# Second matrix chain: output also from seven products of halves, with sums made in PSUM

## The reference

```python
def _moe_ref(x, w_in, w_out):
    h = np.maximum(x @ w_in, 0.0)
    return (h * h @ w_out).astype(np.float32)      # this is y below

def _moe2_ref(x, w1, w2, w3, w_out):
    a = x @ w1                                     # 512 -> 1024
    b = x @ w2
    h = a * b @ w3                                 # 1024 -> 1024
    return (h @ w_out).astype(np.float32)          # 1024 -> 512
```

## Time and profile before

| | |
|---|---|
| median of 3 runs | 1226.66 us (1224.62 to 1226.89) |
| profiled execution | 1226.94 us, span 1225.2 us |
| TensorE busy | 1216.7 us, 99% |
| VectorE busy | 787.5 us, 64% |
| ScalarE busy | 479.3 us, 39% |
| DMA | 183.27 MB, mean 150 GB/s |
| mean granted clock of TensorE | 0.999 |

### The profile page before, as it was taken

The page is one execution under the profiler, slowest core; times in us unless marked ns, Lnnn a source line. Parts: engine busy times, 40 slices in busy tenths (PEclk is TensorE's granted clock), DMA queues, the critical chain, the costliest instruction groups (busy, mean ns, idle before and its releaser), DMA issues.

```text
span 1225.2 us, 16114 instructions
## 1 busy us (share of the span) xinstructions
PE 1216.7 (99%) x5842; PEld 1015.1 (83%) x5842; DVE 787.5 (64%) x1242; ACT 479.3 (39%) x867; POOL 75.5 (6%) x108
## 2 busy tenths in 40 slices
PE   9999999999999999999999999999999999999999
PEld 6677878888888888888888988888888888888888
DVE  6877868677786866667544667656664666465541
ACT  6666555555565554445444431121113111311110
POOL 0001112021121200000000000000000000000000
PEclk9999999999999999999999999999999999999999
DMA  9967664354445422122121463525442554343302
GB/s 316 340 237 254 216 221 138 122 172 139 148 138 176 130 86 94 60 86 69 65 72 51 183 250 137 180 95 223 146 155 95 224 182 153 118 166 137 120 1 86
DMA packets 57613, 183.27 MB, mean 150 GB/s; under 512 B 5200, under 2 KB 6736, under 8 KB 53456
## 3 DMA queue, kind: packets, MB, share of 16 engines
q1 hardware_dynamic: 45088, 137.90, 32.2%
q0 software_dynamic: 12464, 44.57, 10.5%
HBM read 128.97 MB, written 53.48 MB: 149 GB/s over the span
## 4 chain that ended last, share of the span: by engine, by line
PE 97%; DVE 1%; DMA 0%; issue 0%; ACT 0%; SPq 0%; DVEq 0%; ACTq 0%
PE ps_y L700 55%; PE ps_h L700 26%; PE ps_t L700 14%; PE ps_h L761 1%; PE ps_t L724 1%; PE ps_y L761 0%; DMA raw<-in_w_T 0%; PE ps_t L761 0%; DVE v_lo L1256 0%; DVE t L1346 0%; SPq L536 0%; DVE X_lo L1256 0%; DVE stage L1364 0%; SPq L530 0%; ACT v_hi L1006 0%
## 5 line engine op out<-in xcount | busy, mean ns | idle before, releaser
L1006 ACT CAST v_hi<-t 128x512 fp32r<-128x512 f32 (+1 forms) x176 | 106.0, 602 | 407.3 <-DVE t L1256 396.0
L700 PE MATMUL ps_y<-v_hi,X_hi 128*128 128x512 f32 (+1 forms) x576 | 219.2, 380 | 0.3 <-DVE v_lo L1256 0.3
L700 PE MATMUL ps_y<-v_lo,X_hi 128*128 128x512 f32 (+1 forms) x576 | 217.8, 378 | 0.0
L700 PE MATMUL ps_y<-v_hi,X_lo 128*128 128x512 f32 (+1 forms) x576 | 217.7, 378 | 0.0
L1256 DVE TENSOR_TENSOR t<-t 128x512 f32<-128x512 f32 (+1 forms) x208 | 135.9, 666 | 92.9 <-ACT t L1104 92.3
L1256 DVE TENSOR_TENSOR v_lo<-t,v_hi 128x512 fp32r<-128x512 f32 (+1 forms) x176 | 117.5, 668 | 79.3 <-ACT v_hi L1006 69.8
L1104 ACT ACTIVATE t<-ps_h 128x512 f32<-128x512 f32 (+1 forms) x144 | 82.7, 574 | 151.2 <-PE ps_h L700 150.6
L1256 DVE TENSOR_TENSOR t<-t,ps_y 128x512 f32<-128x512 f32 x112 | 76.2, 687 | 76.8 <-PE ps_y L700 76.1
L700 PEld LDWEIGHTS ps_y<-v_hi,X_lo 128*128 128x128 f32 x576 | 108.5, 188 | 20.3
L700 PEld LDWEIGHTS ps_y<-v_hi,X_hi 128*128 128x128 f32 x576 | 108.7, 189 | 20.0 <-issue 0.7
L700 PEld LDWEIGHTS ps_y<-v_lo,X_hi 128*128 128x128 f32 x576 | 108.7, 189 | 19.4
(11 more groups left out here) (255 smaller groups left out, 2273.7 us busy)
## 6 DMA issues: line engine op xcount, KB each, us to landing
top<-s_scratch SPq DMA_DIRECT2D x16, 1792.0 KB, 7.3
s_odd<-s_scratch SPq DMA_DIRECT2D x16, 1792.0 KB, 7.3
raw<-g_scratch SPq DMA_DIRECT2D x64, 256.0 KB
raw<-in_moe_w_in SPq DMA_DIRECT2D x32, 256.0 KB
raw<-in_x_T SPq DMA_DIRECT2D x32, 256.0 KB
raw<-in_x_tok SPq DMA_DIRECT2D x32, 256.0 KB
y_scratch<-stage POOLq DMA_DIRECT2D x8, 1024.0 KB, 6.4
s_scratch<-top POOLq DMA_DIRECT2D x32, 256.0 KB, 3.0
```

The lines of the kernel that those rows point to most:

```text
L700: mm = nc.tensor.matmul(dst, w, m, start=first and n == 0, stop=last and n == 2)
L1006: return nc.scalar.copy(dst, src)
```

## The change

The sums are made of W as well: tiles 5 and 6 get the `S_part` that tiles 1 to 4 have, now on W, and its results go to a new scratch `w_scratch`. W is no longer resident; its seven sums (1.05 MB each) are loaded for every double tile (`load_W`) into three buffers in turn: those of parts 0 to 2 behind the load of chunk 2's sums, those of parts 3 to 6 during the output phase, each when the part three before it is done.

A double tile is now eight chunks one behind the other, without output chunks between them, and then an output phase of seven parts (`out_part`), each 2 x 4 x 3 matmuls of 512 columns: halves of the outputs, of the inner 1024 and of the tokens. v stays in float32 (`e_raw`) over the whole double tile. Sets 1 to 6 of the tokens' side of the output are sums of v (`T_v_pair`, `set_src`) that are split in the output phase, two halves at a time; set 0 is split during the chunks.

In chunks and output alike the order of the products is now 0, 1, 3, 2, 4, 6, 5, and the last three are not added by VectorE: VectorE writes u4 and u3 into the PSUM banks of products 5 and 7, and the last three products are accumulated there onto P1, u4 and u3 (`start` is false for them, `p >= 4`). TensorE waits before them until P1 is copied out, u4 is written, and c22 is read. Per chunk this leaves VectorE u2, u4, u3, c22 and the two multiplications, and gives ScalarE three copies (P1, P5, c11).

The token sets' work of the next double tile (`set_round`, `set_lower`) moves into the output phase between the sets of v. The output is stored in four pieces of 0.5 MB. The remainder's last product takes W from four further loads at the end.

The diff, cut to its core:

```diff
+    w_dram = nc.dram_tensor("w_scratch", [KINDS, P, 4, 2, H], F32, kind="Internal").ap()
...
+        seq = (0, 1, 3, 2, 4, 6, 5)
+        P1_bank, P6_bank, P7_bank, P5_bank = range(4)
+        bank_of = (P1_bank, P6_bank, P5_bank, P7_bank, P1_bank, P5_bank, P7_bank)
...
+        U2, U4, U3, C22, V1, V0, REST = range(1, 8)
...
+        def set_src(p, k, n=2):
+
+            if p in (1, 6):
+                return T24_v[:, k:k + n, :]
+            if p == 2:
+                return T1_rows(k, n)
+            h, s = {0: (0, 0), 3: (0, 1), 4: (1, 0), 5: (1, 1)}[p]
+            return v_rows(h, s, k, n)
...
+        out_of = (0, 1, 3, 2, 0, 3, 2)
...
+            def load_W(t, p):
+                c = N_SETS * t + p
+                if c >= 3:
+                    sp.wait_ge(out_prod, out_count(0, c - 3))
+                sp.dma_start(W_buf(c).bitcast(F32), w_dram[seq[p]].rearrange("p k s n -> p (k s n)")
+                             ).then_inc(W_loaded[c % 3], 16)
...
+                if m == 1:
+                    for p in range(3, N_SETS):
+                        load_W(t - 1, p)
                 load_S(n)
-                t, m = n // KG, n % KG
+                if m == 2:
+                    for p in range(3):
+                        load_W(t, p)
                 if m == 2 and t < TILES - 1:
                     load_y(t + 1)
...
+            def ab_part(n, p):
+
                 t, m = n // KG, n % KG
-                pe.wait_ge(S_loaded[n % 2], 16 * (n // 2 + 1))
...
+                if p == 4:
                     pe.wait_ge(P1_copied, n + 1)
-                else:
-                    pe.wait_ge(prod_used, products_before(n) + used_at[j])
+                if p == 5:
+                    pe.wait_ge(prod_used, used_before(n) + U4)
+                if p == 6:
+                    pe.wait_ge(prod_used, used_before(n) + C22)
+                for kk in range(2):
+                    mm = product(ab_bank(n, bank_of[p]), S_buf[n % 2][:, j, kk, 0], S_buf[n % 2][:, j, kk, 1],
+                                 B_hi[j][:, kk], B_lo[j][:, kk], kk == 0 and p < 4, kk == 1, p >= 4)
+                mm.then_inc(prod_done, 1)
...
-            def out_chunk(t, half, m):
-                pe.wait_ge(ab_split, 2 * (KG * t + m) + half + 1)
...
-                w_hi, w_lo = G(m)
-                for o in range(KM):
-                    cols = slice(o * P, (o + 1) * P)
-                    last = product(out_bank(t, half, o), w_hi[:, cols], w_lo[:, cols], *v_part(half, m),
-                                   m == 0, m == KG - 1)
-                last.then_inc(out_acc, 1)
...
+            def out_part(t, p):
+
+                c = N_SETS * t + p
+                pe.wait_ge(W_loaded[c % 3], 16 * (c // 3 + 1))
...
+                for o in range(2):
+                    if p == 4:
+                        pe.wait_ge(out_P1_copied, 2 * t + o + 1)
+                    if p == 5:
+                        pe.wait_ge(out_u4, 2 * t + o + 1)
+                    if p == 6:
+                        pe.wait_ge(c22_staged, 2 * t + o + 1)
+                    for k in range(4):
+                        if o == 0 and p == 0:
+                            pe.wait_ge(B11_ready, 4 * t + k + 1)
+                        elif o == 0 and k % 2 == 0:
+                            pe.wait_ge(v_set_ready, 2 * ((N_SETS - 1) * t + p - 1) + k // 2 + 1)
+                        w = W_in(c)[:, k]
+                        cols = slice(o * P, (o + 1) * P)
+                        last = product(out_acc_bank(out_of[p], o), w[:, 0, cols], w[:, 1, cols],
+                                       set_part(p, 0, k, 1)[:, 0], set_part(p, 1, k, 1)[:, 0],
+                                       k == 0 and p < 4, k == 3, p >= 4)
+                    last.then_inc(out_prod, 1)
...
-                add(u3, u2, 2)
-                add(u4, u2, 3)
...
+                add(ab_bank(n, P5_bank), u2_in, P5_bank)
+                if between is not None:
+                    between()
+                dve.wait_ge(prod_done, base + 4)
+                add(ab_bank(n, P7_bank), u2_in, P7_bank)
+                dve.wait_ge(prod_used, used + U3)
+                add(c22_in, p5_in, P7_bank)
...
-                for half in range(2):
-                    hi, lo = v_part(half, m)
-                    minus(lo, v_new[half], hi, ab_hi, 2 * n + half + 1, ab_split)
...
+            def out_phase(t):
+                def v_set(p):
+                    for half in range(2):
+                        k = 2 * half
+                        minus(set_part(p, 1, k), set_src(p, k), set_part(p, 0, k), v_set_hi,
+                              2 * ((N_SETS - 1) * t + p - 1) + half + 1, v_set_ready)
...
+            first_block(5, S, slot5, h_of(6, S), slot6, (2, 0))
+            first_block(6, S, slot6, h_of(7, S), tile7_slot, (2, 1))
```

More of the change, by code:

```diff
@@ L577, in _ @@
                 tile(2 * i + 2, tile_slots, R_1 + PT, i, 1)
-            for b in range(NB - 3, NB - 1):
-                tile(b, tile_slots, R_1 + (b - 1) * PT)
+            sp.wait_ge(wp_stored, 16 * 2)
+            for kk in range(2):
+                for n, piece in enumerate(flat(tile_slots)):
+                    load_piece(R_1 + (4 + kk) * PT + n, piece, 5 + kk)
+                    if n == 3:
+                        sp.wait_ge(S_split, 2 * 2 * KINDS + kk * KINDS + 1)
+                        for dst, row, col in ((A11, 0, 0), (A12, 0, 1), (A21, 1, 0), (A22, 1, 1)):
+                            sp.dma_start(dst.rearrange("p (e n) -> p e n", e=2), W_block(kk, row, col)
+                                         ).then_inc(A_loaded, 16)
             tile(7, tile7_slots, R_7)
@@ L695, in passes, with product @@
                 return (w_hi, m_hi), (w_hi, m_lo), (w_lo, m_hi)
-            def product(dst, w_hi, w_lo, m_hi, m_lo, first, last):
+            def product(dst, w_hi, w_lo, m_hi, m_lo, first, last, onto=False):
                 for n, (w, m) in enumerate(passes(w_hi, w_lo, m_hi, m_lo)):
-                    mm = nc.tensor.matmul(dst, w, m, start=first and n == 0, stop=last and n == 2)
+                    mm = nc.tensor.matmul(dst, w, m, start=first and n == 0, stop=last and n == 2,
+                                          skip_group_check=onto)
                 return mm
@@ L973, in first_ab @@
                     pe.wait_ge(relu_done, KF * SR + KF)
-                    ab_chunk(0)
+                    for p in range(3):
+                        ab_part(0, p)
             h0 = batch_h(0, 0, g0_ready)
@@ L993, in _ @@
             first_block(SR, NT, sread_h, no_wait, no_wait, first_ab)
+            for p in range(3, N_SETS):
+                ab_part(0, p)
+            pe.wait_ge(y_drained_act, 2 * (SR + 1))
+            pe.wait_ge(y_drained_dve, 2 * (SR + 1))
             for t in range(TILES):
@@ L1214, in second_block @@
                         ab_chunk(KG * t + m)
[L1215 to L1219 removed]
+                out_phase(t)
             act.wait_ge(g_stored[0], stored(0, STEPS))
@@ L1478, in ab_chunk @@
-                tt(v_new[1], c22, c12, ALU.mult).then_inc(ab_done, 1)
-                for half in range(2):
-                    hi, lo = v_part(half, m)
-                    minus(lo, v_new[half], hi, ab_hi, 2 * n + half + 1, ab_split)
+                dve.wait_ge(prod_done, base + 6)
+                dve.wait_ge(prod_used, used + C22)
+                if t > 0 and m < 2:
+                    dve.wait_ge(v_set_ready, 2 * (N_SETS - 1) * t)
+                tt(v_f(m, 1), c22_in, ab_bank(n, P5_bank), ALU.mult).then_inc(prod_used, 1)
```

503 lines of the change are left out of this document (315 added, 188 removed).

## The result

The changed kernel takes 1229.52 us (median of 11 runs, 1228.25 to 1232.16) against 1225.04 us (11 runs, 1224.62 to 1226.89): ratio 1.0034, 95% interval 1.0025 to 1.0043, 4.5 us slower. The prediction was 1231.2 us. With more runs the median of the kernel before moved from 1226.66 to 1225.04 us; the profiled execution of before, at 1226.94, was one of its slower ones (1.5 us of it lie in the first two tiles, where the changed kernel's trace is that much shorter).

The account below looks back on a forecast made before the run. TensorE was taken to bound the kernel and never wait in the double tiles. From 1226.9 us, - 21.8 (matmuls) + 19.5 (waits) + 0.5 (store) + 6.3 (clock) gave 1231.4, adjusted by 0.3 to 1231.2; range 1218 to 1240 us.

Parts of the forecast that it names:

- 24 matmuls fewer per double tile, 21.8 us: Output of 1024 tokens: 168 matmuls instead of 192, 5.44 us less in each of four double tiles.
- Tiles 5 and 6 carry the sums of W for nothing: First half: making the product matrix's sums in tiles 5 and 6 costs 0; without cover, 8 us.
- The accumulation is in time, and PSUM writes cost 0.69 us: Chunks: u4, c22 and P1's copy ready by 1.1 us at the least, a PSUM-writing addition taken at 0.69 us.
- Chunk 3's sums late by 6.5 us, three times, 0.5 more at t = 0: Chunk 3 at t = 0, 1, 2: TensorE waits for its sums, 19.5 us in all, plus 0.5 us.
- term of the store at t = 0: First double tile: the store of the remainder's y slows chunk 3's sums, charged 0.5 us.
- two figures that I had quoted: DMA ceilings: 435 GB/s for the 16 engines, about 358 GB/s for a core's HBM share; waits near 4.5 or 8 to 9 us.
- The clock: Behind each of chunk 3's three waits TensorE restarts slowly, losing 2.1 us a time, 6.3 us in all.
- The output phase without waits: Output phase: VectorE busy 31.1 of 38.1 us, cost 0, little to spare, tightest at set 3.
- The reason given for the wait: SyncE's queue: chunk 3's sums stand behind all other loads, 8.91 MB, served in order, landing at 25.5 us.
- The clock stays: Rival behind chunk 3's waits: waits come but TensorE resumes at full pace, 1224.9 us; chance 0.20.
- The loads keep up: Rival at chunk 3's sums: loads keep up wholly or in part, 1204.9 us without waits; chance 0.18.
- VectorE becomes the bound: Rival in output phase or accumulation: VectorE late by 9 + 3 us, 1243 us; chance 0.12.

Follow-up runs that it names:

- experiment 1: Changed kernel with the three weight loads behind chunk 2's sums issued one each behind the sums of chunks 3, 4 and 5: 1203.91 us, ratio to before 0.9826.
- experiment 6: Kernel with spread weight loads, product 4's accumulation undone in the chunks: it starts its bank afresh and VectorE adds it to P1; 1203.30 us, ratio 0.9813.
- experiment 2: Changed kernel with only the next tokens' load (2.10 MB) issued behind chunk 3's sums in place of chunk 2's: 1207.84 us, ratio to before 0.9859.
- experiment 3: Changed kernel with only the third of the three weight loads (1.05 MB) moved behind chunk 4's sums: 1220.34 us, ratio to before 0.9960.
- experiment 7: Kernel with spread weight loads, subtraction for the first half of each of sets 1 to 6 done twice in the output phase: 1208.37 us, ratio 0.9857.
- Experiment 5: Changed kernel with its three early weight loads issued by ScalarE, on another queue, behind its copy of chunk 1's P1: 1230.37 us, ratio to before 1.0038.
- experiment 8: Kernel with spread weight loads, subtractions for both halves of each of sets 1 to 6 done twice in the output phase: 1232.46 us, ratio 1.0058.

## Why the prediction was right, point by point

- **24 matmuls fewer per double tile, 21.8 us.** Shown: experiment 1, which is the whole change with three loads moved, is 21.1 us faster than the kernel before by the medians, and from the end of chunk 0 to the end of the span 484.6 us against 506.5 (21.9). The second double tile takes 114.24 us where it took 119.68, the 5.44 us forecast.
- **Tiles 5 and 6 carry the sums of W for nothing.** Right by the trace, 71.60 and 71.87 us. Not tried by itself.
- **The accumulation is in time, and PSUM writes cost 0.69 us.** Right: 0.697 us, and no wait before any product; experiment 6 shows that there is room for a ninth operation.
- **Chunk 3's sums late by 6.5 us, three times, 0.5 more at t = 0.** 18.1 us listed for 20.0: 5.99, 6.26 and 5.88 (19.0 with the 0.3 us that each wait costs beyond its row). The term of the store at t = 0 was 0.5 too much, there was no extra; and the engines ran at 415 GB/s or somewhat more. Experiments 2 and 3 take bytes away from before the sums: 2.10 MB shorten a wait by (18.1 - 2.9) / 3 = 5.1 us, 1.05 MB by (18.1 - 11.1) / 3 = 2.3 us, where 415 GB/s gives 5.1 and 2.5. The two figures that I had quoted from the Trainium skill's page "DMA: Bandwidth & Descriptors" lie to both sides of it.
- **The clock.** 7.0 to 7.2 us measured for 6.3 (the 8.0 of my expectations held the unlisted part of the waits). I had taken 2.1 us a time from the kernel's first matmuls; it is 2.3 to 2.4. That the first matmuls of the kernel and those behind a wait cost about the same was a guess that held; nothing in the trace of before had shown it. The rule of the Trainium skill that I named ("TensorE: Matmul & The Clock Gate", section on HAM oscillation) holds here for the waits of about 6 us: granted clock 0.50 behind each, and 7.1 us back by keeping TensorE busy. Behind the waits of up to 1.3 us in experiment 2 the clock stayed.
- **The total.** The waits were put too high by 1.0 us and the clock too low by 0.7: 26.3 us were charged and 26.1 measured. That they cancel so well is luck. The forecast of 1231.2 us lies 1.7 us above the median because it started from 1226.7 us; as a difference it was 4.5 us, and 4.5 us were measured.
- **The output phase without waits.** Right in the result, and VectorE's 31.1 us of 38.1 were 30.6. "With little to spare" was right too, but I had no number for it: experiment 7 shows that six more operations of 1.2 us are already too many. My expectations there, with 27 us, were worse than the prediction.
- **The reason given for the wait.** I wrote that the sums stand behind 8.91 MB in their queue. Experiment 5 shows that taking 3.15 MB of it to another queue does not help. The bytes issued ahead were the right quantity; that they must be in the same queue was wrong.
- **The rivals.** "The clock stays" fell by the 0.50 rows. "The loads keep up" did not come by itself, but is what experiment 1 makes true, at 1203.9 us against the 1204.9 worked out for it. "VectorE becomes the bound" is what experiment 8 forces; in the changed kernel it does not occur.

## What to carry to other kernels

A change that takes work away from the engine that bounds also moves deadlines closer: here the chunks went from 12.24 to 9.52 us apart at the same moment at which 3.15 MB of loads came in, and together they cost 26.1 us against the 21.8 saved. In numbers, for the second double tile and counted from the end of chunk 0: before, chunk 3's sums landed at 18.0 us and were wanted at 21.8; now they land at 25.2 and are wanted at 19.0. The 3.15 MB account for 7.2 us and the closer chunks for 2.7, and 3.7 us of slack were there, which gives the 6.2 us. By these numbers, as an estimate, the bytes alone would have made 3.5 us of wait and the closer chunks alone none. Add up the bytes that must land before each deadline and divide by the rate of a full stretch of the trace; if it does not fit, move a load before believing the matmul count. A wait of TensorE of several microseconds costs its length and the slow matmuls behind it, here 1.6 to 2.6 us for waits of 3.4 to 6.3 us.

## What the runs showed of the hardware that I had not expected

- Loads issued on two queues share the engines so that neither is spared: with 3.15 MB on ScalarE's queue the tokens landed 20.3 us after issue instead of 18.7, and chunk 3's sums took 15.5 instead of 15.7.
- After waits of 3.44 and 3.95 us TensorE resumed at full pace and slowed down one to three matmuls later, for a loss of 1.6 us each; after 3.69 us it was slow from the first matmul, for 2.6 us, and so it was after 5.88 to 6.26 us, for 2.3 to 2.4 us. After 0.7 to 1.3 us it did not slow down at all.
- A wait costs TensorE about 0.3 us more than its row, even where the clock stays.
- Three times 24 matmuls whose result is thrown away made the kernel 7.1 us faster.
